# Unequal column chunks (452 and five of 512, in place of six of 502) in a transform and two feed-forward layers on one core

## What is computed

```python
X = np.fft.fft(np.fft.fft(x, axis=1), axis=2).real      # x: (2, 3008, 256)
x = X.reshape(6016, 256)
h = x @ moe_w_in;  x = (h * sigmoid(h)) @ moe_w_out     # 256 -> 2048 -> 256
h = x @ moe2_w_in; y = (max(h, 0) + alpha * min(h, 0)) @ moe2_w_out
```

## Time and profile before

| | |
|---|---|
| three runs, us | 933.08, 934.04, 954.89; median 934.04 |
| the profiled execution | 933.09 us, its span 931.2 us |
| granted clock of TensorE over the span | 0.999 |
| busy: TensorE | 923.3 us, 99% of the span |
| busy: VectorE, ScalarE, GpSimd | 635.2, 551.6, 594.4 us |
| DMA | 43 GB/s over the span |

### The profile page before, as it was taken

The page is one execution under the profiler, slowest core; times in us unless marked ns, Lnnn a source line. Parts: engine busy times, 40 slices in busy tenths (PEclk is TensorE's granted clock), DMA queues, the critical chain, the costliest instruction groups (busy, mean ns, idle before and its releaser), DMA issues.

```text
span 931.2 us, 11837 instructions
## 1 busy us (share of the span) xinstructions
PE 923.3 (99%) x4034; PEld 757.2 (81%) x4034; DVE 635.2 (68%) x967; ACT 551.6 (59%) x858; POOL 594.4 (64%) x408
## 2 busy tenths in 40 slices
PE   9999999999999999999999999999999999999998
PEld 4588887788888888888888888888888888888886
DVE  6879996455545545544877777777777777778774
ACT  4575654567667656676665565465555555555544
POOL 0496555259959859676697476566747756664443
PEclk9999999999999999999999999999999999999999
DMA  9512100020020120100300200020020002001001
GB/s 361 222 56 68 45 1 1 1 67 23 13 78 23 55 80 1 45 1 1 124 11 1 71 20 1 0 89 1 1 88 1 1 1 89 1 1 44 1 1 45
DMA packets 19826, 40.35 MB, mean 43 GB/s; under 512 B 1803, under 2 KB 15669, under 8 KB 18741
## 3 DMA queue, kind: packets, MB, share of 16 engines
q1 hardware_dynamic: 18980, 39.05, 11.9%
q10 hardware_dynamic: 688, 0.52, 0.2%
q0 software_dynamic: 96, 0.02, 0.0%
HBM read 27.22 MB, written 12.37 MB: 43 GB/s over the span
## 4 chain that ended last, share of the span: by engine, by line
PE 94%; DVE 2%; POOL 1%; DMA 1%; ACT 1%; issue 0%; SPq 0%; DVEq 0%; ACTq 0%; POOLq 0%
PE ps L354 12%; PE ps L352 12%; PE ps L353 12%; PE ps L668 9%; PE ps L671 9%; PE ps L667 9%; PE ps L613 9%; PE ps L609 9%; PE ps L610 9%; DMA x_tile<-x_tiles 1%; PE ps L556 1%; POOL gl L1313 1%; PE ps L541 1%; PE ps L537 1%; POOL wo L1248 0%
## 5 line engine op out<-in xcount | busy, mean ns | idle before, releaser
L1335 POOL TENSOR_TENSOR gl<-g,gh 128x502 fp32r<-128x502 f32 x192 | 224.8, 1178 | 175.3 <-ACT gh L857 175.3
L1313 POOL TENSOR_TENSOR gl<-g_sb,gh 128x1004 fp32r<-128x1004 f32 x96 | 210.3, 2190 | 121.2 <-ACT g_sb L814 119.2
L851 ACT ACTIVATE g<-ps 128x502 f32<-128x502 f32 x192 | 111.9, 591 | 110.3 <-DVE ps L1196 105.3
L1148 DVE SCALAR_TENSOR_TENSOR h_sb<-n_all,a,v_sb 128x502 f32<-128x502 f32 x96 | 83.1, 865 | 135.1 <-ACT v_sb L876 135.0
L1203 DVE SCALAR_TENSOR_TENSOR g<-g,less_alpha,ps 128x502 f32<-128x502 f32 x192 | 132.6, 732 | 31.9 <-ACT g L851 31.8
L609 PE MATMUL ps<-gh,wo 128*128 128x502 f32 x384 | 148.8, 388 | 0.3
L610 PE MATMUL ps<-gh,wo 128*128 128x502 f32 x384 | 147.9, 385 | 0.0
L667 PE MATMUL ps<-gh,wo 128*128 128x502 f32 x382 | 147.3, 386 | 0.0
L668 PE MATMUL ps<-gh,wo 128*128 128x502 f32 x382 | 147.3, 386 | 0.0
L857 ACT CAST gh<-g 128x502 fp32r<-128x502 f32 x192 | 113.0, 614 | 40.3 <-DVE g L1203 38.6
L876 ACT COPY v_sb<-ps 128x502 f32<-128x502 f32 x96 | 55.6, 580 | 122.5 <-PE ps L354 118.4
(11 more groups left out here) (132 smaller groups left out, 1618.4 us busy)
## 6 DMA issues: line engine op xcount, KB each, us to landing
x_tile<-x_tiles SPq DMA_DIRECT2D x6, 1024.0 KB, 13.5
x_rows<-x SPq DMA_DIRECT2D x6, 1004.0 KB, 5.9
out_t<-out_sb SPq DMA_DIRECT2D x11, 502.0 KB, 3.2
x_raw_b<-x_rows SPq DMA_DIRECT2D x18, 251.0 KB, 4.0
stage<-moe_w_out SPq DMA_DIRECT2D x16, 256.0 KB, 4.5
n_parts<-n_rows SPq DMA_DIRECT2D x5, 502.0 KB, 3.7
stage<-moe_w_in SPq DMA_DIRECT2D x8, 256.0 KB, 5.0
w_sb<-moe_w_in SPq DMA_DIRECT2D x3, 512.0 KB, 7.8
```

The lines of the kernel that those rows point to most:

```text
L851: act.activation(g4[:, k, :], product_bank(u, TILE_IN[k]), ACT.Relu, scale=-1.0).then_inc(relu_done, 1)
L1313: pool.tensor_tensor(gl[g % 2][:, :, :], g_sb[g % 2][:, :, :], gh[g % 2][:, :, :].bitcast(F32), ALU.subtract).then_inc(gl_done, 1)
L1335: pool.tensor_tensor(gl4[:, k, :], g4[:, k, :], gh4[:, k, :].bitcast(F32), ALU.subtract).then_inc(gl_done, 1)
```

## The change

The columns of both sequences are one run of 3,012, cut into a first chunk of 452 and five of 512. `WIDTHS` and `STARTS` take the place of `N`, and every operation on a chunk runs over its own width. Chunk 3 begins with the last 30 columns of sequence 0 (`FROM_0`). Its place in `pq` can't be written at that time, so these columns go to a tile `hold`, and after sequence 1's transforms `n_hold_round` and `n_hold_low` bring them in. Chunk 3 to 5 now wait for `t23_lo` to be complete, where 4 and 5 did. Tiles that were N wide are 512 wide, and the rows of the DRAM tensors too; the output tensor is one row of columns.

```diff
-N = COLS // 3
 ROW = 512
-NC1 = 3 * BATCH
-NC2 = 2 * NC1
+NC1 = -(-BATCH * COLS // ROW)
+WIDTHS = [BATCH * COLS - ROW * (NC1 - 1)] + [ROW] * (NC1 - 1)
+STARTS = [sum(WIDTHS[:c]) for c in range(NC1 + 1)]
+FIRST = [0, 3]
+FROM_0 = COLS - STARTS[FIRST[1]]
...
-def cut(at, width):
-    out, done = [], 0
-    while done < width:
-        c, o = divmod(at + done, N)
-        w = min(width - done, N - o)
-        out.append((c, o, done, w))
+def cut(b, blk):
+    at, out, done = b * COLS + BLOCK_AT[blk], [], 0
+    while done < BLOCK_W[blk]:
+        c = max(i for i in range(NC1) if STARTS[i] <= at + done)
+        w = min(BLOCK_W[blk] - done, STARTS[c + 1] - at - done)
+        out.append((c, at + done - STARTS[c], done, w))
         done += w
...
+        hold = at("hold", XS_AT + 8192, [P, 2, FROM_0], F32)
...
             bank = pair_at(g)
-            return ps[:, bank:bank + 2, 0:N]
+            return ps[:, bank:bank + 2, 0:WIDTHS[g // NF]]
...
-                    if c in (4, 5):
+                    if c >= 3:
                         pe.wait_ge(t23_lo, len(T23_JOBS))
...
-                for c, o, a, w in cut(BLOCK_AT[blk], BLOCK_W[blk]):
+                for c, o, a, w in cut(b or 0, blk):
                     if s == "n":
-                        ins = act.copy(pq[0:1, c, 2, o:o + w], ps[0:1, bank, a:a + w])
+                        dst = pq[0:1, c, 2, o:o + w] if c < 3 else hold[0:1, 1, :]
+                        ins = act.copy(dst, ps[0:1, bank, a:a + w])
                     else:
-                        ins = act.copy(pq[:, 3 * b + c, 2 * (s == "q"), o:o + w], ps[:, bank, a:a + w])
+                        dst = pq[:, c, 2 * (s == "q"), o:o + w] if c < 3 or b else hold[:, int(s == "q"), :]
+                        ins = act.copy(dst, ps[:, bank, a:a + w])
...
             def n_hold_round():
                 act.wait_ge(t23_lo, t23_of(3, 1, "q"))
+                act.copy(pq[:, 3, 0:4:2, 0:FROM_0], hold[:, :, :])
...
             def n_hold_low():
                 dve.wait_ge(t23_hi, len(T23_JOBS))
+                dve.tensor_tensor(pq[:, 3, 1:4:2, 0:FROM_0], hold[:, :, :], pq[:, 3, 0:4:2, 0:FROM_0].bitcast(F32),
+                                  ALU.subtract)
...
-    out_t = nc.dram_tensor("out_t", (D, NC2, N), F32, kind="ExternalOutput").ap()
+    out_t = nc.dram_tensor("out_t", (D, 2 * BATCH * COLS), F32, kind="ExternalOutput").ap()
```

More of the change, by code:

```diff
@@ L153, in build @@
         assert XS_AT + 8192 + 2 * ROW * 4 <= STAGE_AT and W1_AT + 14 * ROW * 4 <= W2_AT
-        xr = [{row: at(f"x_{row[0]}_{row[1]}_{i}", place, [P, N], F32R) for row, place in X_PLACE[i].items()} for i in range(2)]
-        xr_raw = [{x: at(f"x_raw_{x}_{i}", X_PLACE[i][x, 1], [P, N], F32) for x in X_ROWS} for i in range(2)]
+        xr = [{row: at(f"x_{row[0]}_{row[1]}_{i}", place, [P, ROW], F32R) for row, place in X_PLACE[i].items()} for i in range(2)]
+        xr_raw = [{x: at(f"x_raw_{x}_{i}", X_PLACE[i][x, 1], [P, ROW], F32) for x in X_ROWS} for i in range(2)]
         stage = [at(f"stage{i}", STAGE_AT + 2048 * i, [P, 512], F32) for i in range(SLOTS)]
@@ L527, in spread_n0 @@
                 for i in range(2):
-                    ins = pe.matmul(ps[:, N0_BANK, 0:N], ones[0:1, :], pq[0:1, 0, 2 + i, :], start=i == 0, stop=i == 1)
+                    ins = pe.matmul(ps[:, N0_BANK, 0:WIDTHS[0]], ones[0:1, :], pq[0:1, 0, 2 + i, 0:WIDTHS[0]], start=i == 0, stop=i == 1)
                 ins.then_inc(n0_pe, 1)
@@ L601, in second1 @@
                     pe.wait_ge(stage_lo, f // 2 + 1)
-                out = [(sg, ft, ps[:, 4 + 2 * sg + ft, 0:N]) for sg in range(2) for ft in range(2)]
+                out = [(sg, ft, ps[:, 4 + 2 * sg + ft, 0:WIDTHS[c]]) for sg in range(2) for ft in range(2)]
                 for sg, ft, dst in out:
@@ L621, in product @@
                 wh, wl = (w7[w][:, i, fp * P:(fp + 1) * P] for i in range(2))
-                xh, xl = (xr[n % 2][x, i][:, :] for i in range(2))
+                xh, xl = (xr[n % 2][x, i][:, 0:WIDTHS[n]] for i in range(2))
                 return three(pe, product_bank(u, p), wh, wl, xh, xl, True, True)
@@ L657, in second2 @@
                 pe.wait_ge(gh_done, STEPS1 + 4 * u + k + 1)
-                out = [ps[:, 4 + 2 * sg + ft, 0:N] for ft in range(2)]
+                out = [ps[:, 4 + 2 * sg + ft, 0:WIDTHS[n]] for ft in range(2)]
+                g_hi, g_lo = (t[:, k, 0:WIDTHS[n]] for t in (gh4, gl4))
                 if (u, k) == (UNITS - 1, 3):
@@ L875, in _ @@
                     act.wait_ge(h_done, g)
-                act.copy(v_sb[:, :], pair(g)[:, 1, :]).then_inc(v_done, 1)
+                act.copy(v_sb[:, 0:WIDTHS[g // NF]], pair(g)[:, 1, :]).then_inc(v_done, 1)
                 if g == 0:
@@ L1092, in t23_low @@
                 bank = t_bank(blk, b, s)
-                for c, o, a, w in cut(BLOCK_AT[blk], BLOCK_W[blk]):
+                for c, o, a, w in cut(b or 0, blk):
+                    if c >= 3 and not b:
+                        continue
                     if s == "n":
@@ L1097, in t23_low @@
                     else:
[L1098 removed]
+                        lane = pq[:, c, :, o:o + w]
                         m = 2 * (s == "q")
@@ L1428, in token_columns @@
                 sign = 1 - sign
-            c, o = divmod(b * COLS + at[k], N)
-            idx[b, s] = (2 * c + sign) * N + o
+            j = b * COLS + at[k]
+            c = max(i for i in range(NC1) if STARTS[i] <= j)
+            idx[b, s] = STARTS[c] + sign * WIDTHS[c] + j
     return idx.reshape(-1)
```

170 lines of the change are left out of this document (89 added, 81 removed).

## The result

The changed kernel takes 937.75 us (median of 6 runs, 937.67 to 938.14) where the kernel before, beside it, takes 933.78: ratio 1.0043, 95% interval 1.0030 to 1.0057. That is no change by the 2% bound, as forecast, but the loss is 4.0 us where 1.85 were forecast, and its interval leaves zero well out. Some executions of a kernel take longer as a whole (one of the first three, 954.89, and those in the traces of e1 and e2), and ratios and differences leave them out, so that of e2's trace only the first layer is read, up to where its matmuls leave the pace of before.

The account below looks back on a forecast made before the run. TensorE's matmuls were taken as the bound. First layer +1.05 us, second layer +0.7 and the rest +0.1 made +1.85, carried from a median of 934.04 to 935.9 us, with an 8-in-10 range of 926 to 941.

Parts of the forecast that it names:

- Rival (b): Chunk 0, both layers: GpSimd and VectorE can't feed it, nothing of 13.5 us won, 947.5 us; chance 0.10.
- one column a cycle: TensorE matmuls: fixed part plus a cycle per column, so 512 columns cost 4.17 ns more, 452 cost 20.8 less.
- any straight line gives the same total: TensorE: columns and matmuls both stay, so whether the 14.1 ns are fixed or grow doesn't matter.
- the uncrowded part of chunk 0: First layer, after the crowded steps: 132 matmuls with slack each save 20.8 ns, 2.75 us.
- (a): TensorE: width is rounded or 502 pays for its ragged end; mild 922.4 us, chance 0.09, strong 898.1, 0.05.
- (c): TensorE: weight loads set the 223.3 ns, so neither width changes anything, 934.1 us; chance 0.08.
- gl falls by a tenth, 0.215: GpSimd, first layer's crowded steps: 452 columns shorten gl by 0.215 us, giving a period of 4.07 us.
- weight split about 1.1: GpSimd's output weight split, a term of the first layer's crowded period, taken as about 1.1 us and unshrunk.
- STT about 0.65: VectorE's SCALAR_TENSOR_TENSOR, a term of the crowded period, about 0.65 us, shrinking by 0.065 with 452 columns.
- the second layer: Its start: TensorE arrives 1.4 us sooner but the x rows' DMA doesn't, 0.7 us lost (ends 0 and 1.5).
- The losses fall where TensorE is never waiting: Wide chunks: the column losses, 6.0 us in the first layer and 7.5 in the second, are paid in full.
- both signs of being wrong: Wrong would be a step in chunk 0 longer than 4.0 us, or TensorE waits beyond 6 us in total.

Follow-up runs that it names:

- e1: Changed kernel with gh, gl and what lies behind them moved up by 64 bytes; 949.6 us, ratio 1.0162.
- e2: Kernel before (six chunks of 502) with its tiles on the changed kernel's addresses, rows of 2,048 bytes; 938.16 us, ratio 1.0041.
- e12: Changed kernel with g written two columns (8 bytes) further on in the narrow chunk alone, no tile moved; 934.43 us, ratio 1.0011.
- e4: Changed kernel with the first layer's gl computed for only 64 columns of each half, the rest zero; 932.35 us, ratio 0.9983.
- e8: Kernel before (502) with g_sb and g4 in rows of 2,016 bytes starting 8 bytes further on; 933.12 us, ratio 0.9999.
- e7: Changed kernel with chunks of 462 and five of 510, rows of 2,040 bytes for g, h, v and n; 936.63 us, ratio 1.0034.
- e6: Changed kernel in e1's layout, with GpSimd subtractions behind its work whose inputs or output are shifted by 4 to 40 bytes; 1.09 us at 8 bytes.
- e3: Changed kernel with matmul bursts of several widths and shifted GpSimd subtractions behind its work; 226.7 ns at 512 columns, 109 to 112 from 192 down.
- e9: Changed kernel with gh and gh4 moved by 8 bytes and what lies behind by 32; 950.9 us, ratio 1.0181.
- e11: Changed kernel with only what lies behind gl (x rows, last weight buffer, small setup tiles) moved up 64 bytes; 940.12 us, ratio 1.0066.

## Why the prediction was right and wrong

**Right: the bound and the main form.** TensorE's matmuls bound the kernel, gains and losses of width cancel, and what decides is whether GpSimd can feed the narrow chunk. The start, from the 64th matmul to the `gl` that was at 47.13, won 0.6 us where 0.4 was forecast (the profiled execution had 0.45 of scatter against it); the copies of the 30 held columns show as 0.17 us of its chain. Rival (b) holds in the crowded steps alone: from 77.8 us on chunk 0 goes at 3.72 us a step.

**Wrong in size: the price of a column.** The step "one column a cycle" gave 4.17 and 20.8 ns; measured are 3.33 and 16.7, and 510 columns cost the same as 512. The argument "any straight line gives the same total" held for the total and hid that the line isn't straight, so that the cancelling was partly luck. It took 0.6 us from the 2.75 that the uncrowded part of chunk 0 was to win (2.17 measured), and gave back 2.7 in the wide chunks of both layers. Of the rivals, (a) as it stands is out, since 512 costs more than 502, though that 510 costs what 512 does is a step of the kind it had in mind; (c) is out, since width does change the pace.

**Wrong: "gl falls by a tenth, 0.215".** This is the step that failed. In the crowded stretch it fell from 2.69 to 2.60, by 0.09; the period went to 4.20 and not 4.07, and the stretch won 0.75 us (27.72 to 26.97) and not 1.7 to 1.8. The prediction scaled by columns, with the half-sized `gl` of 1.07 us in the earlier trace rows as proof that nothing is fixed. That row was one of the fast kind. The group's mean, 1178 ns against 2190 for twice the elements, was on the page, and 1.07 beside a mean of 1.18 should have led to a search for the other kind. Beyond that, the new rows (2,008 bytes become 2,048) stood in the diff, and the layout got no term. e12 gives the size of such a term, from all pairs alike to all apart: 2.5 us in the first layer's chunk 0 and some 0.5 in the second's. Nor were the other terms of the period read: "weight split about 1.1" takes 1.30 us where GpSimd is not held up (e4), and "STT about 0.65" 0.74 (the rows shown with e8); with the fold's 0.67 the four make 4.9, so that the 4.35 was matched and not derived.

**Right in number, in part by luck: the second layer.** It cost 0.83 us where 0.7 was forecast, for x rows that come late by DMA. The stops that came are in three of its first units, 0.1 to 0.2 us each, and e12, with the same DMA, has none of them: they were the slow `gl`'s.

**Missing: the wide chunks' own waits.** "The losses fall where TensorE is never waiting" is wrong for the steps in which the second layer's weights are made. There GpSimd is full too. The kernel before stopped in three such steps for 0.2 us each, and the prediction did not look for them; in the changed kernel the stops are 0.4 to 0.5 us longer (the one ahead of 226.90 is the first), and two hand-overs between chunks 0.2 us longer: 1.9 of the 2.2 us. e4 shows that they are GpSimd's, since with a short `gl` they are gone. That most of it is the slower `gl` and not the 2% more columns is shown by two runs: in e2, with 502 columns and all pairs alike, the three stops are 0.3 us longer than before, and in e7, with 510 columns and every other pair apart, they and the hand-overs are no longer than before. What 452 and 512 take with all pairs apart and TensorE undisturbed was not measured.

The sum, by the same steps: forecast -0.4, -1.8, -2.75, +6.0, +0.7, +0.1 = +1.85; measured -0.58, -0.75, -2.17, +6.98, +0.83, and +0.45 for the late start, = +4.76; without the last 4.3, beside 4.0 by the medians. By the prediction's own signs: steps of 4.08 and 3.72 us came for 4.10 and 3.65; chunk 1 began 3.1 us earlier and not about 5, the second layer 3.9 us later and not about 1; and both signs of being wrong came, steps of chunk 0 over 4.0 us (which the forecast 4.07 had already allowed) and waits over 6 us.

**The rules cited.** The port pair that VectorE and GpSimd take in turn was the prediction's ground for a period as a sum. The traces bear it out as far as they go: in e12, with `gl` 0.35 us shorter in the crowded stretch, the SCALAR_TENSOR_TENSOR beside it is 0.4 to 0.9 shorter, and the same instruction takes 0.74 us in the kernel before, where it starts ahead of GpSimd's, and 1.74 in e8, where it starts behind it. The Trainium skill, SBUF — State Buffer, section Operand start alignment, says where an operand may start and adds "This is about legality, not speed", and that its runs timed nothing. Here it is about speed as well: 1.09 against 1.29 us for one subtraction, by 8 bytes. The Trainium skill, TensorE: Matmul & The Clock Gate, section Back-to-back issue gap, gives N/2.4 + 2.5 ns for a single matmul by itself, 215.8 at 512 columns, and about 131 ns for a sustained stream with weight loads at 512. The fp32r matmuls here, each with a weight load of its own, agree with neither: 226.7.

## What to carry to other kernels

Before you price an instruction by its size, compare the single row with its group's mean and look for two kinds of it; where they alternate, find out what alternates with them. Compare two traces from an event behind the first DMAs: their landing moved everything by up to 1.2 us here, where 4 us were in question. A change of widths or row pitch is a change of addresses too: list which tiles start at new bytes and which instructions read two of them. And where an engine feeds a chunk that you make shorter, its cost has to fall with it, or its spare time is what you spend.

## What the runs showed of the hardware

- GpSimd's subtraction of two 128x512 f32 inputs in SBUF takes 1.26 to 1.30 us when the start of the first less that of the second is 0 or 4 bytes modulo 16 and 1.09 when it is 8 or 12. The output's start and shifts of both inputs together don't matter (e6), nor do shifts by multiples of 32 bytes (e3).
- A SCALAR_TENSOR_TENSOR of VectorE on 128x502 in SBUF takes 0.74 us when it starts just before an SBUF-only instruction of GpSimd, which then takes 1.81 us, and 1.74 when it starts just behind one, which takes 1.30 (before, e8).
- An fp32r matmul with a weight load of its own, at the granted clock of 1.00 (2.4 GHz), starts 206.7 ns after the last at 452 columns, 211.6 at 462, 223.3 at 502 and 226.7 at both 510 and 512; from 192 columns down it stays at 109 to 112 (e3).
- These prices hold for the layout of both kernels. Moving TensorE's operands by as little as 8 and 32 bytes (e9) made the 512-column matmuls 232, moving them by 64 bytes 230.5 (e1's layout in e6); those of 452 columns stayed at 206 to 207 in all of these. In e11 only the last tiles moved, by 64 bytes. Of the moved x rows the matmuls on `x_t` went to between 227 and 237 ns and those on `x_b` stayed at 226.7; those that read `gh`, which had not moved, went to 227.4 in chunks 1, 3 and 5 and to 230.4 in chunks 2 and 4, while `gl`'s stayed at 226.8. So it isn't the moved operand alone, and it isn't the distance to a multiple of 64. Which pair of addresses it takes stays open; the cost of getting it wrong here is 2 to 18 us, which can be more than the change itself.
